# Products with the decay state, split per head onto quarters of the TensorE array, in a linear-attention and two-layer kernel

## The reference

```python
B, H, S, D = 4, 8, 768, 48
state = zeros((B, H, D, D))
for t in range(S):
    state = alpha[:, :, t, :, None] * state + einsum('bhd,bhe->bhde', k[:, :, t], v[:, :, t])
    y[:, :, t] = einsum('bhd,bhde->bhe', q[:, :, t], state)
x = y.transpose(0, 2, 1, 3).reshape(B * S, H * D)
x = (sigmoid(x @ w_gate) * (x @ w_val)) @ w_out            # d_ff 1536
x = maximum(maximum(x @ w1, x @ w2), x @ w3) @ w_out2      # d_ff 768
```

## Time and profile before

| | |
|---|---|
| median of 3 executions | 880.43 us (879.71 to 882.51) |
| profiled execution: time, span | 880.59 us, 878.8 us |
| TensorE matmul (PE) busy | 852.8 us, 97% |
| TensorE weight load (PEld) busy | 796.1 us, 91% |
| VectorE (DVE), ScalarE (ACT), GpSimd (POOL) busy | 372.2, 286.6, 122.7 us |
| DMA | 42.17 MB, 48 GB/s on average |

### The profile page before, as it was taken

How to read it: one execution, slowest core, us unless ns; L and a number is a source line. 1 busy time by engine, 2 the same in 40 slices (tenths; PEclk the granted TensorE clock), 3 DMA queues, 4 the chain that set the end, 5 groups by cost and what they waited for, 6 DMA issues and landing times.

```text
span 878.8 us, 13847 instructions
## 1 busy us (share of the span) xinstructions
PE 852.8 (97%) x5405; PEld 796.1 (91%) x5405; DVE 372.2 (42%) x722; ACT 286.6 (33%) x566; POOL 122.7 (14%) x97
## 2 busy tenths in 40 slices
PE   5689999999999999999999999999999999999997
PEld 4689999999999999999999999988888888888886
DVE  8555465375365356356455432232323232232321
ACT  3355433333333333334333334321212122131211
POOL 5156321021011011011011104400000000000000
PEclk9799999999999999999999999999999999999999
DMA  7350200201111011021021022200000000000001
GB/s 302 97 208 1 97 32 16 95 5 45 48 50 46 24 73 46 5 92 45 4 95 45 1 79 73 72 1 1 36 1 1 36 0 36 0 36 0 36 0 39
DMA packets 14452, 42.17 MB, mean 48 GB/s; under 512 B 1984, under 2 KB 5952, under 8 KB 14400
## 3 DMA queue, kind: packets, MB, share of 16 engines
q1 hardware_dynamic: 14336, 41.38, 13.4%
q10 hardware_dynamic: 64, 0.05, 0.0%
HBM read 35.52 MB, written 4.72 MB: 46 GB/s over the span
## 4 chain that ended last, share of the span: by engine, by line
PE 96%; DVE 1%; ACT 1%; POOL 1%; DMA 0%; issue 0%; ACTq 0%; SPq 0%; POOLq 0%
PE ps_out L916 17%; PE ps_val L891 17%; PE ps_gate L891 17%; PE ps_gate L897 9%; PE ps_val L897 8%; PE ps_out L996 6%; PE ps_sc L891 6%; PE ps_sc L849 3%; PE ps_y L880 3%; PE ps_sc L897 3%; PE ps_y L876 2%; PE ps_sc_odd L996 2%; PE ps_y L833 1%; PE ps_sc L859 1%; DMA inbuf<-att_in 0%
## 5 line engine op out<-in xcount | busy, mean ns | idle before, releaser
L891 PE MATMUL ps_gate<-x_hi,w_hi 128*128 128x384 f32 (+1 forms) x396 | 139.8, 353 | 2.5 <-ACT w_hi L393 1.9
L891 PE MATMUL ps_val<-x_hi,w_hi 128*128 128x384 f32 (+1 forms) x396 | 140.8, 355 | 0.0
L891 PE MATMUL ps_gate<-x_hi,w_lo 128*128 128x384 f32 (+1 forms) x396 | 139.1, 351 | 0.0
L891 PE MATMUL ps_val<-x_hi,w_lo 128*128 128x384 f32 (+1 forms) x396 | 138.8, 350 | 0.0
L897 PE MATMUL ps_gate<-x_lo,w_hi 128*128 128x384 f32 (+1 forms) x396 | 118.3, 353 | 2.2 <-DVE x_lo L664 2.2
L693 DVE TENSOR_TENSOR h_sb<-act_sb,ps_val 128x384 f32<-128x384 f32 x96 | 52.7, 549 | 156.3 <-PE ps_val L897 156.2
L897 PE MATMUL ps_val<-x_lo,w_hi 128*128 128x384 f32 (+1 forms) x396 | 117.2, 350 | 0.0
L393 ACT ACTIVATE h_hi<-h_sb 128x384 fp32r<-128x384 f32 x96 | 50.4, 525 | 150.0 <-DVE h_sb L693 150.0
L435 ACT ACTIVATE act_sb<-ps_gate 128x384 f32<-128x384 f32 x96 | 47.2, 492 | 128.2 <-PE ps_gate L897 128.2
L801 DVE TENSOR_TENSOR probs<-probs,ps_val 128x512 f32<-128x512 f32 x36 | 24.7, 686 | 137.8 <-PE ps_val L897 137.8
L897 PEld LDWEIGHTS ps_gate<-x_lo,w_hi 128*128 128x128 f32 x396 | 73.4, 189 | 7.8 <-DVE x_lo L664 2.7
(11 more groups left out here) (103 smaller groups left out, 1297.0 us busy)
## 6 DMA issues: line engine op xcount, KB each, us to landing
inbuf<-att_in SPq DMA_DIRECT2D x23, 704.0 KB, 5.4
mid<-w SPq DMA_DIRECT2D x12, 576.0 KB, 7.1
inbuf<-att_in SPq DMA_DIRECT2D x23, 256.0 KB, 3.1
inbuf<-w SPq DMA_DIRECT2D x6, 768.0 KB, 4.3
out<-inbuf SPq DMA_DIRECT2D x5, 768.0 KB, 3.5
x_raw<-y_last SPq DMA_DIRECT2D x46, 24.0 KB, 1.9
out<-inbuf SPq DMA_DIRECT2D x4, 192.0 KB, 2.5
mid<-att_in SPq DMA_DIRECT2D x1, 704.0 KB, 8.8
```

The lines of the kernel that those rows point to most:

```text
L891: mm(bank, w_at(half, f, c + k * P, total=total), x_hi[:, k, 0:w], start=(k == 0 and half == 0), stop=False)
```

## The change

The state products become one per head. `state` keeps only the 48 by 48 blocks, both heads of a pair in the same 48 columns, each on its own partitions. A product of L876 reads its head's rows (0 to 47 or 64 to 111, a row half of the array) and writes y on a column half chosen by `y_slot`. So its part of the array is a quarter. Head `n` of pair `p` goes to bank `n`, to partitions 0 to 47 or 64 to 111 by `(p + n) % 2`, and to slot `p // 2` there. y now stands in the last two slots of one bank and the first two of the next. These banks are those of the transposes (`ps_tr`) and of `ps_sc_odd`, which lie next to each other as `ps_pair`; the bank `ps_y` is gone. A column half now holds heads of both kinds, so the order of the features in `x_raw` is another (`head_at`, and the rows of the first layer's weights on the host follow it).

What goes with it:

- `scores` waits for the copy of the chunk before (`y_evac`), in the start too, because `ps_sc_odd` holds y.
- `y_copy` is two instructions of 48x512 instead of four (48x128 and 48x384 twice each). `y_last` is the fourth slot of `x_raw`. Chunk 2 alone keeps the four.
- `new_state` is one add and one multiply on 112 partitions instead of two each on 48.
- `outer` writes both heads of a pair to the same 48 columns.
- `move_last` waits for `y_evac`.

```diff
-        x_raw = sb("x_raw", [P, KT, TOK])
+        x_raw = sb("x_raw", [P, PAIRS, TOK])
-        state = sb("state", [P, 2, PAIRS, PR])
+        state = sb("state", [P, 2, PAIRS, D])
-        y_last = sb("y_last", [P, TOK])
-        ps_sc_odd = pb("ps_sc_odd", [P, 512])
-        ps_y = pb("ps_y", [P, PAIRS, CH])
+        ps_pair = pb("ps_pair", [P, 2 * 512])
+        ps_tr, ps_sc_odd = ps_pair[:, 0:512], ps_pair[:, 512:1024]
+        ps_y = ps_pair[:, 512 - 2 * CH:512 + 2 * CH].rearrange("p (s t) -> p s t", s=PAIRS)
+        y_last = x_raw[:, KT, :]
...
             def y_copy(Cs, i):
-                for r in HALVES:
-                    ins = copy(y_last[r, t], ps_y[r, KT, :])
-                ins.then_inc(last_evac, 1)
-                for r in HALVES:
-                    ins = copy(x_raw[r, :, t], ps_y[r, 0:KT, :])
-                ins.then_inc(y_evac, 1)
...
+                else:
+                    copy(x_raw[HALVES[0], :, t], ps_y[HALVES[0], :, :])
+                    copy(x_raw[HALVES[1], :, t], ps_y[HALVES[1], :, :]).then_inc(y_evac, 1)
...
             def new_state(Cs, i):
-                for n, r in enumerate(HALVES):
...
+                u = outer_bank(Cs, i)[0:PR, 0:PAIRS * D].rearrange("p (a e) -> p a e", a=PAIRS)
...
+                    nc.vector.tensor_tensor(stmp[0:PR], u, state[0:PR, cur], ALU.add).then_inc(stmp_done, 1)
...
+                    nc.vector.tensor_tensor(state[0:PR, new], stmp[0:PR], end, ALU.mult).then_inc(state_done, 1)
...
             def scores(Cs, i):
                 if not (isinstance(i, int) and Cs == 0):
                     pe.wait_ge(mask_done, 2 * C)
+                    pe.wait_ge(y_evac, C)
...
+            def y_slot(p, n):
+
+                return ps_y[HALVES[(p + n) % 2], 2 * n + p // 2, :]
...
             def attend(Cs, i):
                     for p in range(PAIRS):
-                        mm(ps_y[0:PR, p, :], state[0:PR, par, p, :], att(buf(Cs), Q)[:, p, :],
-                           start=(p == 0), stop=False, skip_group_check=True)
+                        for n, r in enumerate(HALVES):
+                            mm(y_slot(p, n), state[r, par, p, :], att(buf(Cs), Q, r)[:, p, :],
+                               start=(p < 2), stop=False, skip_group_check=True)
                 for p in range(PAIRS):
-                    for n, r in enumerate(HALVES):
-                        ins = mm(ps_y[r, p, :], v_cols(buf(Cs), (2 * p + n) * D, D), probs[:, PAIRS * n + p, :],
-                                 start=(first and p == 0), stop=True, skip_group_check=True)
+                    for n in range(2):
+                        ins = mm(y_slot(p, n), v_cols(buf(Cs), (2 * p + n) * D, D), probs[:, PAIRS * n + p, :],
+                                 start=(first and p < 2), stop=True, skip_group_check=True)
```

More of the change, by code:

```diff
@@ L55, with head_at @@
 RING = 8
+def head_at(half, s):
+    n, j = s // 2, s % 2
+    return 2 * j + (half + n) % 2, n
 def build(nc, att_in, vT, w1, w2, consts, y, out):
@@ L166, in u_bank @@
                 return ps_out[:, 1, :]
-            return ps_y.rearrange("p a t -> p (a t)")
+            return ps_tr
         def outer_bank(Cs, i):
@@ L236, in move_last @@
             def move_last(T, parts=range(KT)):
-                sp.wait_ge(last_evac, CPT * (T + 1))
+                if isinstance(T, int) and T == 0:
+                    sp.wait_ge(y_evac, CPT - 1)
+                    sp.wait_ge(last_evac, 1)
+                else:
+                    sp.wait_ge(y_evac, CPT * (T + 1))
                 for k in parts:
@@ L279, in slow_layers @@
                             for r in (0, 1):
+                                (p, n0), (pl, nl) = head_at(r, k), head_at(r, KT)
                                 for n, (row, src) in enumerate((
-                                        (ODD * r, y[b * PAIRS + k, r, :, half * TOK:(half + 1) * TOK]),
-                                        (ODD * r + D, y[b * PAIRS + KT, r, GAP * k:GAP * (k + 1),
+                                        (ODD * r, y[b * PAIRS + p, n0, :, half * TOK:(half + 1) * TOK]),
+                                        (ODD * r + D, y[b * PAIRS + pl, nl, GAP * k:GAP * (k + 1),
                                                         half * TOK:(half + 1) * TOK]))):
@@ L412, in y_copy @@
                 t = slice(c * CH, (c + 1) * CH)
-                for r in HALVES:
-                    ins = copy(y_last[r, t], ps_y[r, KT, :])
-                ins.then_inc(last_evac, 1)
-                for r in HALVES:
-                    ins = copy(x_raw[r, :, t], ps_y[r, 0:KT, :])
-                ins.then_inc(y_evac, 1)
+                if isinstance(i, int) and Cs == CPT - 1:
+                    for r in HALVES:
+                        ins = copy(y_last[r, t], ps_y[r, KT, :])
+                    ins.then_inc(last_evac, 1)
+                    for r in HALVES:
+                        ins = copy(x_raw[r, 0:KT, t], ps_y[r, 0:KT, :])
+                    ins.then_inc(y_evac, 1)
+                else:
+                    copy(x_raw[HALVES[0], :, t], ps_y[HALVES[0], :, :])
+                    copy(x_raw[HALVES[1], :, t], ps_y[HALVES[1], :, :]).then_inc(y_evac, 1)
             def x_split(T, k, src, n=TOK):
@@ L532, in _ @@
             y_copy(2, 0)
-            act.wait_ge(last_evac, CPT)
+            act.wait_ge(y_evac, CPT - 1)
+            act.wait_ge(last_evac, 1)
             for r in (0, ODD):
@@ L648, in new_state @@
                 dve.wait_ge(end_done, C + 1)
-                for n, r in enumerate(HALVES):
[L650 to L657, removed]
+                u = outer_bank(Cs, i)[0:PR, 0:PAIRS * D].rearrange("p (a e) -> p a e", a=PAIRS)
+                end = d_end[0:PR, cur, :].rearrange("p (a e) -> p a e", e=1).broadcast_to([PR, PAIRS, D])
+                if Cs % (2 * CPT) == 0:
+                    nc.vector.tensor_tensor(state[0:PR, new], u, end, ALU.mult).then_inc(state_done, 1)
+                else:
+                    dve.wait_ge(state_done, C)
+                    nc.vector.tensor_tensor(stmp[0:PR], u, state[0:PR, cur], ALU.add).then_inc(stmp_done, 1)
                     later = Cs - Cs // (2 * CPT) - 1 + 5 * i
-                    dve.wait_ge(stmp_done, 2 * later + n + 1)
-                    nc.vector.tensor_tensor(state[r, new, :, e], stmp[r, :, :], end, ALU.mult).then_inc(state_done, 1)
+                    dve.wait_ge(stmp_done, later + 1)
+                    nc.vector.tensor_tensor(state[0:PR, new], stmp[0:PR], end, ALU.mult).then_inc(state_done, 1)
             def x_rest(k, n, src, w=TOK):
@@ L830, in transposes @@
                 elif Cs > 0:
-                    pe.wait_ge(state_done, 2 * C)
+                    pe.wait_ge(state_done, C)
                 for p in range(PAIRS):
@@ L1100, in lay_out @@
         for r in range(2):
-            order += [(2 * t + r) * D + e for e in range(D)]
-            order += [(2 * KT + r) * D + GAP * t + e for e in range(GAP)]
+            for (p, n), lo, rows in ((head_at(r, t), 0, D), (head_at(r, KT), GAP * t, GAP)):
+                order += [(2 * p + n) * D + lo + e for e in range(rows)]
     def lhs(w, nf):
```

8 lines of the change are left out of this document (4 added, 4 removed).

## The result

The changed kernel takes 879.23 us (median of 16 runs, 878.31 to 880.30), the kernel before 881.45 in the same comparison (16 runs, 879.71 to 883.20). The ratio is 0.9976, with a 95% interval of 0.9969 to 0.9982: faster by 0.24%, which is clear of noise, and less than the 0.3% that the prediction called no change. The profiled executions stand at 878.90 and 880.59 us, with spans of 877.1 and 878.8.

What follows compares the result with a forecast made beforehand. PE was taken as the bound from 51 to 511 us, the start as a chain across engines. 880.6 - 5.3 (steady part) + 0.8 (start) + 1.0 (clock) = 877.1, less 0.2 for the median: 877.0 us; range 874.3 to 886.0.

Steps and rivals of the forecast that it cites:

- State products, 5.3 us less: Steady part: 16 quarter records, four in a step, cost 0.58 us a chunk against 0.87; 18 chunks save 5.3 us.
- The price taken for one more cut of the array: State products: going from quarters to column halves once more per chunk costs 0.08 to 0.09 us.
- The halves' order costs nothing: L880's records in column-half order 0,1,1,0 cost nothing; the rival that they cost 9 us had chance 0.05.
- No new wait lies behind the start: Steady part: `scores` waiting for `y_evac` costs nothing, the 1.2 us copy being asked for some 6 us earlier.
- Waits before `scores`: Start: scores wait for 1.19 us copies of y, coming 1.4 us later in chunk 1 and 1.3 in chunk 2.
- Chunk 1's state products 0.9 less: Start, chunk 1: at half rate, the state products take 1.1 us instead of 1.98, 0.9 less.
- Chunk 2's 0.3 less: Start, chunk 2: the state products, taken at full rate, cost 0.3 us less.
- `x_lo` 0.7 sooner: Start, first tile: two `new_state` instructions ahead of `x_lo` go, so it comes 0.7 us sooner.
- The clock, 1.0 of 0 to 3: Start: waits before both `scores` may delay TensorE's clock rise, costing 0 to 3 us; 1.0 was taken.
- two at a time: Rival on state products: quarters sharing rows or columns take turns, 8 steps, 1.00 us a chunk, 886.0 us; chance 0.17.
- five steps: Rival on state products: program-order starts give steps of 2, 4, 4, 4, 2 records, 879.1 us; chance 0.10.
- The want of feeding: Rival: TensorE's sequencer brings records too slowly, a chunk costs 0.76 us, total 880.4 us; chance 0.08.

Runs made afterwards that it cites:

- e8: The changed kernel run once more unaltered, on the chip of e7, for a second profile of its start: 879.46 us, ratio 0.9977.
- e3: The changed kernel with four products that nothing reads before the scores of chunks 1 and 2, waits kept: 875.41 us, ratio 0.9933.
- e1: The changed kernel with y of chunks 0 to 2 in the unused gate and value banks, so scores need not wait: 874.57 us, ratio 0.9926.
- e4: The changed kernel with the state products in the order of pairs 0, 2, 1, 3: 879.34 us, ratio 0.9981.
- e7: e1 with products that nothing reads in TensorE's other waits of the start, nine more before attend of chunk 1: 871.41 us, ratio 0.9890.

## Why the prediction was wrong in size

The sum made the kernel 3.5 us faster than its own profiled execution (880.6 to 877.1). The two profiled executions are 1.7 apart and the medians 2.2; the measured 879.23 is 2.2 above the forecast 877.0 and inside its range. Of these 2.2 us 1.0 is the base: the forecast started from 880.43, the median of three executions of the kernel before, and that of 16 is 881.45. The other 1.2 are the change: by ratio the forecast was 0.9961 and the result 0.9976. Step by step:

- **State products, 5.3 us less: right.** Four records in a step, 0.585 us from the first to L901 against 0.58 forecast, 0.289 saved in a chunk, 18 x 0.289 = 5.2 (as is 18 x 0.29; the 5.3 of the sum was a slip of 0.1). The price taken for one more cut of the array (0.09) fits that sum.
- **Not in the sum: the products behind.** L937's nine products behind an attend with a state take 63.82 to 65.51, 1.69 us, against 60.84 to 62.51, 1.67, before. That is 0.02 a chunk, 0.4 in all. It is so behind each of the 18 attends with a state, while behind the three without one the changed kernel has 1.67 as before; so it goes with the state products on quarters. The rest of the span is 5.0 shorter in one profile and 5.6 in the other, too coarse to confirm so small a term. The quarters leave PE's instruction stream a little behind, I suppose; the trace doesn't show the cause.
- **The halves' order costs nothing: right**, 0.91 us from L901 to L875 as before. No new wait lies behind the start: right.
- **Waits before `scores`.** The copies take 1.20 us (1.19 forecast), and the scores of chunk 1 come 1.6 us later (1.4 forecast), counted from L880 or L901 of chunk 0 (14.20 and 14.54). For chunk 2 I counted 1.3 more, and they came 1.9 later: 1.60 of wait, and 0.3 because L901 of chunk 1 stayed at half rate to its end. That is already the clock.
- **Chunk 1's state products 0.9 less: right** (0.94). **Chunk 2's 0.3 less: wrong.** At half rate they take 1.11 us to record, and those of before took 1.13 at full rate: nothing is gained. **`x_lo` 0.7 sooner: right** (0.9 less waiting).
- **The clock, 1.0 of 0 to 3: the step that failed, in its size.** I took the case in between, because a rise at 24 us had stood behind 3.7 us of work without a wait, and I could not tell what 1.5 us of idle time would do to it. It did all it could: no rise before 43.78. Chunk 1's L901 cost 0.3 us by it. From the scores of chunk 2 to those of chunk 3 the changed kernel takes 26.74 us and in e8 26.86, against 26.28 before, where the forecast without its clock term had 1.0 less (0.3 and 0.7 of the points above): 1.5 to 1.6 more. Together that is 1.8 to 1.9 us in place of 1.0, inside the bound of 3. It is measured against one profile of the kernel before, whose executions differ by more than that. The 3.8 us of e3 are another quantity, since its clock rises 6 us sooner than in the kernel before; they show what the clock can cost, not what this change lost by it.

Against e1, which has no such waits and whose clock rises at 25.63 (so it has the 0.3 of chunk 1 too), the changed kernel's start is 4.1 us longer (4.7 in the second profile and by the medians). Between e8 and e1 it is 1.6 up to the scores of chunk 1, 1.6 from there to those of chunk 2, both about the waits, and 1.5 from there to those of chunk 3, the clock. The forecast had 1.4, 1.3 and 1.0 for the three terms, 3.7 in all.

The start was forecast at +1.8 us in all and came to +2.3 in one profile and +3.0 in the other, the fairer one; the rest was forecast at -5.3 and came to -5.0 and -5.6. The lower end of the range, 874.3, lies a little below what the forecast's own best case gives (880.6 - 5.3 - 0.5 - 0.2 = 874.6).

The rivals: two at a time is refuted by the counts of 4, 8 and 12 in the narrow stretches, and so are five steps, whose counts would be 2, 6, 10. The Trainium skill, page "TensorE: Matmul & The Clock Gate", section "The mechanism", has matmuls start strictly in program order. The trace of e4 disagrees, as far as its four starts per step let one infer it: the fifth and sixth product start ahead of the third and fourth. The want of feeding isn't there for the quarters themselves (16 records in 0.585 us), and at most in the 0.02 behind them. Section "Back-to-back issue gap" of the same page of the Trainium skill gives 62 ns per matmul where firmware decodes them. By that 16 records would take 0.99 us, an estimate; the trace has 0.585.

## What to carry to other kernels

A wait added to TensorE in a stage where engines take turns costs more than its length: price the work behind it at half rate as well, and look for the rise of the clock that it may put off. Here two waits, 3.1 to 3.2 us in sum, made the kernel 4.7 us slower than e1 and turned a gain of some 6.5 us (e1's ratio) into 2.2. When buffers are merged, give the first rounds a bank that nobody uses yet, or fill the wait with products that nothing reads: both together took some 8 us off the changed kernel for a few lines (e7 871.41, e8 879.46, on one chip).

## What the runs showed of the hardware

- Added TensorE work made the kernel faster by 3.8 us (e3: the waits stayed, and the first rise of the clock came at 17.95 in place of 43.78) and, with the free banks, by some 8 (e7 against e8).
- Quarters of the array run fully beside each other in fp32: 16 records of 48x48 by 128 columns start in four steps, 0.15, 0.11 and 0.11 us apart, in both orders of the pairs that were tried. The step is 0.11 for 128 columns at full rate whether records cover the whole array, halves or quarters.
- The clock of a stretch ahead of the first recorded change reads 1.00 where the rows of single instructions are at half rate: 1.11 us in place of 0.65 for the same 16 records. The time of a known instruction is the better witness.
